# Product 4 of an up quad issued behind product 6 of the next quad

## The chip, the cores and the metric

The kernel runs on one core of one Trainium2 chip. The metric is the device time of one launch in microseconds (us). Three runs of the kernel before gave 1362.82, 1363.51 and 1364.30 us, a median of 1363.51 us.

## What is computed

Attention over 2 batches, 8 heads and 768 positions; then a dense layer pair with a sigmoid-weighted activation; then 8 experts, each a layer pair with a plain rectifier, mixed by weights that 8 rounds of row and column normalisation make even.

```python
def _moe_ref(x, w_in, w_out):            # x 1536x512, w_in 512x2048, w_out 2048x512
    h = x @ w_in
    g = h * (1.0 / (1.0 + np.exp(-h)))
    return g @ w_out

def _moe2_ref(x, w_gate, w1, w2):        # w1 8x512x1024, w2 8x1024x512
    logits = x @ w_gate
    P = np.exp(logits - logits.max())
    for _ in range(8):
        P /= P.sum(1, keepdims=True) + 1e-09
        P /= P.sum(0, keepdims=True) + 1e-09
        P *= N / E
    for e in range(E):
        out += P[:, e:e + 1] * (np.maximum(x @ w1[e], 0.0) @ w2[e])
```

## The kernel before

**Steps.** After attention, which ends about 104 us into the span, the work is 20 steps. A step is one batch (768 tokens) with one block of 1024 hidden columns. Steps 0 to 3 are the dense pair (two blocks for each of two batches, called the silu steps here), steps 4 to 19 are the 8 experts for batch 0 and then for batch 1 (the relu steps). Step 4 (`GATE`) also carries the gate: logits, their largest value, and the rounds of normalisation.

**Quads.** A step has four quads, i = 0 to 3, and then `down`. A quad makes two blocks of 128 hidden columns for both halves of the tokens out of seven products instead of eight: `RECIPE` names for each product the slot of the weights (a sum or difference of quarters) and the slot of the inputs. Each fp32 operand is split into a high and a low part (`up_h`, `up_l`, `xc_h`, `xc_l`), so that `multiply` issues six matmuls of 384 columns for each product: two halves of the depth times high-high, low-high and high-low. Names such as P6(3) below mean product 6 of quad 3.

**Banks.** P1 and P2 add up in a bank called a, P5 and P3 in c, P6 and P7 in b (two of each, used in turn by even and odd quads), and P4 in the single bank d. Between the products ScalarE copies partial sums: `keep_p1` copies a into b (P6 adds onto that copy, so `p6` waits for it), `keep_p5` copies c to SBUF, `keep_u2` copies b to SBUF after P6 (P7 waits for it), `keep_u3` copies b into d after P7 (P4 of that quad waits for it). VectorE adds the two remaining sums (`add12` after P3, `add22` after `keep_u3`).

**Order on TensorE before.** In a quad with i > 0: P1(i), P5(i), P4(i-1), P6(i), P2(i), P3(i), P7(i). Quad 0 has no P4, and P4(3) stands in `down`, in the first tile. P1(0) and P5(0) of the next step stand in the last tile of `down`.

**Order on ScalarE and VectorE.** Both work through queues that are written out by hand. ScalarE (`quad_work`): `keep_p1(i)`, `hidden22(i-1)`, `keep_p5(i)`, `hidden21(i-1)` (which waits for P4(i-1)), a rounding of new weights (`split_up` or `split_down`, L946, L956), `keep_u2(i)`, `hidden11(i)` (waits for P2), a second rounding, `hidden12(i)` (waits for `add12`), `keep_u3(i)`, a third rounding. VectorE: `hidden22(i-1)`, `hidden21(i-1)`, low part of the first rounding, `hidden11(i)`, low part of the second, `add12(i)`, `hidden12(i)`, `add22(i)`, low part of the third. In a relu step a hidden function is one instruction on each (L1013 and L1384); in a silu step it is one on ScalarE (L1019) and two on VectorE (L1390 and L1392).

**Weights just in time.** In quad i = 2 the weights of quad 3 are split, in three pieces (`PIECES`): slots 0 to 2, 3 and 4, 5 and 6. P1 uses slot 0, P5 slot 4, P4 slot 2, P6 slot 5, which is in the third piece: ScalarE rounds it behind `keep_u3(2)` and VectorE subtracts behind `add22(2)`. Quads 0, 1 and 2 of a step have theirs from the `down` before. In step 4, VectorE runs `rows_even` and `round_on` between the hidden functions of quads 2 and 3, each round waiting for a column sum of TensorE (`token_sums`), which waits for the step before it.

The counts that the waits on `product` use come from the table `made`, which lists the products in TensorE's order.

Of the kernel before, what the change touches and what calls it, by code (L numbers as in the profile page):

```python
# [29 lines left out]
def mixture_kernel(nc, qT, kT, v, vg, sizes, w_up, w_down, w_gate, out):  # L30
# [5 lines left out]
    NBLK, FP, _, _ = w_up.shape  # L36
# [18 lines left out]
    with ExitStack() as whole:  # L55
# [213 lines left out]

        made = {}  # L270
        for quad in range(QUADS):
            for name in ("P1", "P5", "P4", "P6", "P2", "P3", "P7"):
                if name != "P4":
                    made[quad, name] = len(made) + 1
                elif quad % FP:
                    made[quad - 1, name] = len(made) + 1
            if quad % FP == FP - 1:
                made[quad, "P4"] = len(made) + 1
# [38 lines left out]
        with nc.Block() as block:  # L317
# [241 lines left out]
            def _(pe):  # L559
# [127 lines left out]
                def multiply(quad, name, ps, add):  # L687
                    w, x = RECIPE[name]
                    s = quad // FP
                    pe.wait_ge(up_ready, len(PIECES) * quad + PIECE_OF[w] + 1)  # L690
                    if quad % FP == 0 and s in turns:
                        pe.wait_ge(xc_ready, SLOTS * turns.index(s) + x + 1)
                    n = 0
                    for k in range(2):
                        for a, b in ((up_h, xc_h), (up_h, xc_l), (up_l, xc_h)):
                            mm = nc.tensor.matmul(ps[:, 0:HALF], a[quad % UP_BUFS][:, w, k, :], b[x][:, k, :],  # L696
                                                  start=(n == 0 and not add), stop=(n == 5), skip_group_check=True)
                            n += 1
                    mm.then_inc(product, 1)

                def p1(s, i):
                    quad = s * FP + i
                    if i >= 2:
                        pe.wait_ge(hid_ready, 4 * (quad - 2) + 1)
                    elif s > 0:
                        pe.wait_ge(acc_ready, outs_before[s - 1] + 3 * i + 1)
                    multiply(quad, "P1", a_ps[i % 2], False)

                def p5(s, i):
                    quad = s * FP + i  # L710
                    if i >= 2:
                        pe.wait_ge(summed, 2 * (quad - 2) + 1)
                    elif s > 0:
                        pe.wait_ge(acc_ready, outs_before[s - 1] + 3 * i + 2)
                    multiply(quad, "P5", c_ps[i % 2], False)

                def p4(quad):
                    pe.wait_ge(kept, 4 * quad + 4)
                    multiply(quad, "P4", d_ps, True)

                def p6(s, i):
                    pe.wait_ge(kept, 4 * (s * FP + i) + 1)
                    multiply(s * FP + i, "P6", b_ps[i % 2], True)

                def p2(s, i):
                    multiply(s * FP + i, "P2", a_ps[i % 2], True)
# [58 lines left out]
                def turn_logits():  # L785
                    pe.wait_ge(gate_kept, 1)
                    place = ident[0:LOGITS, 0:32 * TB].rearrange("p (b r) -> p b r", r=32)[:, :, 0:E]
                    for n in range(WIDE):
                        mm = nc.tensor.matmul(g_ps[:, n * TB * E:(n + 1) * TB * E], logits_kept()[:, n * P:(n + 1) * P], place,
                                              start=True, stop=True)  # L790
                    mm.then_inc(gate_done, 1)
# [24 lines left out]
                def second_part():  # L816
                    for s in range(STEPS):
                        for i in range(FP):
                            if i > 0:
                                p1(s, i)  # L820
                                p5(s, i)
                            if s == GATE and i == 1:
                                turn_logits()
                            if i > 0:
                                p4(s * FP + i - 1)
                            if s == GATE and i == 2:
                                token_sums(0)
                            if s > 0 or i > 0:
                                p6(s, i)
                            if s == GATE and i == 1:  # L830
                                turn_top()
                            p2(s, i)
                            p3(s, i)
                            if s == GATE and i == 1:
                                spread_top()
                            p7(s, i)
                            if s == GATE and i == 0:
                                logits()
                            elif s == GATE and i > 1:
                                token_sums(i - 1)  # L840
                        down(s, {j: (lambda it=j + 2: token_sums(it)) for j in range(1, 6)} if s == GATE else {})
# [811 lines left out]
```

## Time and profile before

| | value |
|---|---|
| median of 3 runs | 1363.51 us |
| the profiled execution | 1364.54 us |
| its span, first to last instruction | 1363.0 us |
| mean granted TensorE clock | 0.998 |
| PE, weight load, VectorE, ScalarE, GpSimd busy | 99%, 90%, 58%, 46%, 24% |
| six L696 matmul groups and L761 groups on the chain that ended last | 38% and 38% of the span |

The busy shares are those of the whole span; matmuls overlap, so PE shows busy also where it only just keeps up. A matmul of 384 columns has a duration of 334 ns, yet the next one starts 0.17 us behind it, so a product of six takes 1.04 us. The same times recur in every relu step, one step being 62 us.

### The profile page before, as it was taken

The page shows a single profiled execution, that of the slowest core. Times are in us where ns is not written, and L with a number is a line of the kernel's source. Part 1 is how long each engine was busy: PE and PEld are TensorE (multiplying, and loading weights), DVE is VectorE, ACT ScalarE, POOL GpSimd, SP SyncE. Part 2 cuts the span into 40 slices and gives each one's busy share as a digit, 9 for nine tenths or more (in the row PEclk, how much of TensorE's full clock was granted, in tenths as well). Part 3 has the DMA queues.
Part 4 walks back from the last instruction along what each step waited for, and adds up shares of the span by engine and source line. Part 5 has one row for each costly group of instructions (what it writes and reads, how often), then busy time and mean ns, then how long its engine had stood idle before and what let it go on. Part 6 is the DMA issues. An engine that isn't in the chain of part 4 may idle for free.

```text
span 1363.0 us, 19886 instructions
## 1 busy us (share of the span) xinstructions
PE 1344.6 (99%) x7326; PEld 1223.8 (90%) x7326; DVE 794.2 (58%) x1444; ACT 620.9 (46%) x1323; POOL 325.6 (24%) x385
## 2 busy tenths in 40 slices
PE   7999999999999999999999999999999999999998
PEld 5779999999889898989898998989898998989896
DVE  6667476848486645546464647646464646455452
ACT  7786263526352533426262535435262535334250
POOL 6452303121311303030312302140313213040200
PEclk9999999999999999999999999999999999999999
DMA  7401212211212212121221212321212212131111
GB/s 240 142 4 55 86 47 85 79 53 57 74 49 85 87 38 93 47 78 47 85 78 55 78 62 70 102 92 47 77 58 82 77 61 91 36 93 47 62 32 63
DMA packets 48675, 98.73 MB, mean 72 GB/s; under 512 B 5313, under 2 KB 14529, under 8 KB 48577
## 3 DMA queue, kind: packets, MB, share of 16 engines
q1 hardware_dynamic: 48576, 97.42, 22.6%
q8 instruction: 62, 1.02, 0.3%
q14 instruction: 37, 0.29, 0.1%
HBM read 94.26 MB, written 3.15 MB: 71 GB/s over the span
## 4 chain that ended last, share of the span: by engine, by line
PE 90%; DVE 5%; ACT 3%; issue 1%; DMA 0%; DVEq 0%; ACTq 0%
PE bank L761 38%; PE bank L696 38%; PE bank L758 10%; ACT prob L876 1%; DVE hid_l L1392 1%; PE bank L572 1%; PE bank L585 1%; DVE hid_h L1390 1%; PE bank L605 1%; DVE up_l L1342 1%; ACT parts L1019 1%; PE bank L616 1%; DVE parts L1372 0%; DVE parts L1377 0%; PE bank L624 0%
## 5 line engine op out<-in xcount | busy, mean ns | idle before, releaser
L696 PE MATMUL bank<-xc_h,up_h 128*128 128x384 f32 x1120 | 375.9, 336 | 1.0 <-DVE up_l L1342 0.4
L696 PE MATMUL bank<-xc_h,up_l 128*128 128x384 f32 x1120 | 375.1, 335 | 0.0
L696 PE MATMUL bank<-xc_l,up_h 128*128 128x384 f32 x1120 | 374.9, 335 | 0.0
L761 PE MATMUL bank<-down_h,hid_l 128*128 128x512 f32 x768 | 299.7, 390 | 0.0
L761 PE MATMUL bank<-down_l,hid_h 128*128 128x512 f32 x768 | 299.6, 390 | 0.0
L761 PE MATMUL bank<-down_h,hid_h 128*128 128x512 f32 x768 | 299.4, 390 | 0.0
L482 POOL TENSOR_TENSOR up_raw<-up_raw 128x256 f32<-128x256 f32 x80 | 69.0, 863 | 896.2 <-DMA up_raw<-w_up 896.2
L1342 DVE TENSOR_TENSOR up_l<-up_raw,up_h 128x512 fp32r<-128x512 f32 (+1 forms) x234 | 200.8, 891 | 49.2 <-ACT up_h L946 49.0
L696 PEld LDWEIGHTS bank<-xc_h,up_h 128*128 128x128 f32 x1120 | 210.3, 188 | 6.8 <-issue 3.2
L696 PEld LDWEIGHTS bank<-xc_l,up_h 128*128 128x128 f32 x1120 | 210.3, 188 | 2.7
L696 PEld LDWEIGHTS bank<-xc_h,up_l 128*128 128x128 f32 x1120 | 210.3, 188 | 0.0
L946 ACT CAST up_h<-up_raw 128x512 fp32r<-128x512 f32 (+1 forms) x240 | 157.4, 687 | 67.8 <-POOL up_raw L487 64.3
L761 PEld LDWEIGHTS bank<-down_h,hid_l 128*128 128x128 f32 x768 | 144.1, 188 | 30.2
L761 PEld LDWEIGHTS bank<-down_l,hid_h 128*128 128x128 f32 x768 | 144.2, 188 | 28.0
L761 PEld LDWEIGHTS bank<-down_h,hid_h 128*128 128x128 f32 x768 | 144.2, 188 | 27.8
L1560 DVE SCALAR_TENSOR_TENSOR x_sb<-bank,mix,x_sb 128x512 f32<-128x512 f32 x84 | 60.0, 751 | 178.1 <-PE bank L761 178.1
L979 ACT COPY bank<-bank 128x384 f32<-128x384 f32 x80 | 37.1, 464 | 269.4 <-PE bank L696 269.4
L956 ACT CAST down_h<-down_raw 128x512 fp32r<-128x512 f32 x160 | 98.9, 618 | 95.5 <-PE bank L761 70.8
L1347 DVE TENSOR_TENSOR down_l<-down_raw,down_h 128x512 fp32r<-128x512 f32 x160 | 125.2, 785 | 27.4 <-ACT down_h L956 27.3
L1384 DVE SCALAR_TENSOR_TENSOR hid_l<-bank,hid_h 128x384 fp32r<-128x384 f32 x128 | 71.3, 558 | 114.0 <-ACT hid_h L1013 114.0
L1384 DVE SCALAR_TENSOR_TENSOR hid_l<-parts,hid_h 128x384 fp32r<-128x384 f32 x128 | 76.1, 595 | 71.2 <-ACT hid_h L1013 69.0
L1013 ACT ACTIVATE hid_h<-parts 128x384 fp32r<-128x384 f32 x128 | 67.1, 524 | 98.8 <-DVE parts L1372 78.4
(119 smaller groups left out, 1484.2 us busy)
## 6 DMA issues: line engine op xcount, KB each, us to landing
up_raw<-w_up SPq DMA_DIRECT2D x80, 512.0 KB, 3.5
down_raw<-w_down SPq DMA_DIRECT2D x160, 256.0 KB, 2.7
k_sb<-kT SPq DMA_DIRECT2D x12, 288.0 KB, 4.5
q_sb<-qT SPq DMA_DIRECT2D x12, 256.0 KB, 3.9
v_sb<-v SPq DMA_DIRECT2D x12, 256.0 KB, 4.5
out<-x_sb SPq DMA_DIRECT2D x12, 256.0 KB, 2.7
vg_sb<-vg SPq DMA_DIRECT2D x2, 256.0 KB, 5.4
nraw<-sizes SPq DMA_DIRECT2D x1, 2.0 KB, 2.8
```

The source lines that it names most:

```text
L482: nc.gpsimd.tensor_tensor(w[4], w[3], w[2], ALU.add).then_inc(up_summed, 1)
L696: mm = nc.tensor.matmul(ps[:, 0:HALF], a[quad % UP_BUFS][:, w, k, :], b[x][:, k, :], start=(n == 0 and not add), stop=(n == 5), skip_group ...
L758: mm = nc.tensor.matmul(ps[:, 0:HALF], w[a][:, t // 2 * P:t // 2 * P + P], x[b][:, t % 2, :], start=start, stop=stop)
L761: mm = nc.tensor.matmul(ps[:], x[a][:, t // 3, t % 3 * P:t % 3 * P + P], w[b], start=start, stop=stop)
L946: nc.scalar.copy(up_h[quad % UP_BUFS][:, lo:hi, :, :], up_raw[:, quad % RAWS, lo:hi, :, :]).then_inc(up_h_ready, 1)
L956: nc.scalar.copy(down_h[:, tile % DOWN_BUFS, :], down_raw[:, tile % RAWS, :]).then_inc(down_h_ready, 1)
L979: nc.scalar.copy(b_ps[i % 2][:, 0:HALF], a_ps[i % 2][:, 0:HALF]).then_inc(kept, 1)
L1013: nc.scalar.activation(hid_h[:, f, half, :], src, ACT.Relu).then_inc(hid_h_ready, 1)
L1342: nc.vector.tensor_tensor(up_l[quad % UP_BUFS][:, lo:hi, :, :], up_raw[:, quad % RAWS, lo:hi, :, :], up_h[quad % UP_BUFS][:, lo:hi, :, :]. ...
L1347: nc.vector.tensor_tensor(down_l[:, tile % DOWN_BUFS, :], down_raw[:, tile % RAWS, :], down_h[:, tile % DOWN_BUFS, :].bitcast(F32), ALU.su ...
L1384: nc.vector.scalar_tensor_tensor(low, src, 0.0, h.bitcast(F32), ALU.max, ALU.subtract).then_inc(hid_ready, 1)
L1560: nc.vector.scalar_tensor_tensor(acc(c, t), part, weight, acc(c, t), ALU.mult, ALU.add).then_inc(acc_ready, 1)
```

## The change

In `second_part`, the call of `p4` for the quad before moves from in front of `p6` to behind it. The order of a quad with i > 0 becomes P1(i), P5(i), P6(i), P4(i-1), P2(i), P3(i), P7(i). The table `made` is changed in the same way, so every wait on a product still means the same product. In step 4, `token_sums(0)` stood behind P4(1) and now stands directly behind P5(2); `turn_top` stood behind P6(1) and now has P4(0) between.

```diff
-            for name in ("P1", "P5", "P4", "P6", "P2", "P3", "P7"):
+            for name in ("P1", "P5", "P6", "P4", "P2", "P3", "P7"):
...
-                            if i > 0:
-                                p4(s * FP + i - 1)
                             if s == GATE and i == 2:
                                 token_sums(0)
                             if s > 0 or i > 0:
                                 p6(s, i)
+                            if i > 0:
+                                p4(s * FP + i - 1)
```

The queues of ScalarE, VectorE, GpSimd and SyncE hold the same instructions in the same order as before. On TensorE, quad 3 of step 5 (every step from 1 on has this pattern, apart from the numbers of the weight buffers): the first of the six matmuls of P1, P5, P4, P6, P2, P3 and P7 before. bank4 is d, bank3 is b, bank5 is a, bank6 is c; up_h1 holds the weights of quad 2, up_h2 those of quad 3.

```order
L696 MATMUL bank5<-xc_h0_62,up_h2_82 128x384 [waits up_ready,hid_ready]
...
L696 MATMUL bank6<-xc_h1_63,up_h2_82 128x384 [waits up_ready,summed]
...
L696 MATMUL bank4<-xc_h6_75,up_h1_107 128x384 [waits up_ready,kept]
...
L696 MATMUL bank3<-xc_h2_64,up_h2_82 128x384 [waits up_ready,kept]
...
L696 MATMUL bank5<-xc_h3_65,up_h2_82 128x384 [waits up_ready]
```

The same place of the changed kernel, on TensorE:

```order
L696 MATMUL bank5<-xc_h0_62,up_h2_82 128x384 [waits up_ready,hid_ready]
...
L696 MATMUL bank6<-xc_h1_63,up_h2_82 128x384 [waits up_ready,summed]
...
L696 MATMUL bank3<-xc_h2_64,up_h2_82 128x384 [waits up_ready,kept]
...
L696 MATMUL bank4<-xc_h6_75,up_h1_107 128x384 [waits up_ready,kept]
...
L696 MATMUL bank5<-xc_h3_65,up_h2_82 128x384 [waits up_ready]
```

P6(3), which reads the third piece of new weights and adds onto the copy of P1, has moved up by one product, and P4(2), for which `hidden21(2)` waits, has moved down by one.

On TensorE, quad 2 of step 4, where the first column sum (L803) stands. Before:

```order
L696 MATMUL bank1<-xc_h1_63,up_h0_72 128x384 [waits up_ready,summed]
...
L696 MATMUL bank4<-xc_h6_75,up_h2_82 128x384 [waits up_ready,kept]
...
L803 MATMUL bank7<-mix_58,ones_54 128x96 [waits gate_step]
L696 MATMUL bank2<-xc_h2_64,up_h0_72 128x384 [waits up_ready,kept]
...
L696 MATMUL bank0<-xc_h3_65,up_h0_72 128x384 [waits up_ready]
```

And in the changed kernel:

```order
L696 MATMUL bank1<-xc_h1_63,up_h0_72 128x384 [waits up_ready,summed]
...
L803 MATMUL bank7<-mix_58,ones_54 128x96 [waits gate_step]
L696 MATMUL bank2<-xc_h2_64,up_h0_72 128x384 [waits up_ready,kept]
...
L696 MATMUL bank4<-xc_h6_75,up_h2_82 128x384 [waits up_ready,kept]
...
L696 MATMUL bank0<-xc_h3_65,up_h0_72 128x384 [waits up_ready]
```

The column sum now has P5(2) in front of it in place of P4(1), and P4(1) (bank4) stands behind both the sum and P6(2).

## Rows read from the trace of the kernel before

**Rows 1.** The page's busy times: us (share of the span) and instructions.

```profile
PE 1344.6 (99%) x7326; PEld 1223.8 (90%) x7326; DVE 794.2 (58%) x1444; ACT 620.9 (46%) x1323; POOL 325.6 (24%) x385
```

**Rows 2.** Waits of PE's weight loads: us in total, times, longest us.

```profile
PEld bank L696 <- ACT bank L1008: 0.7, 2, 0.4
```

**Rows 3.** The chain that ended last: start us, us, what, instructions.

```profile
233.36 9.37 PE bank L696 x54
...
259.78 1.56 PE bank L758 x9
...
429.68 26.02 PE bank L696 x150
...
1297.30 26.02 PE bank L696 x150
```

**Rows 4.** Timeline of PE, step 6: first matmul of P4(2). Start, us, what.

```profile
512.31 0.33 PE L696 MATMUL bank<-xc_h,up_h 128*128 128x384 f32 x1
```

**Rows 5.** Timeline of ScalarE, step 6, quads 2 and 3; brackets: idle before, releaser.

```profile
504.19 0.46 ACT L979 COPY bank<-bank 128x384 f32<-128x384 f32 x1
...
506.27 0.49 ACT L1013 ACTIVATE hid_h<-bank 128x384 fp32r<-128x384 f32 x1 [0.47 <-PE bank L696]
506.65 0.83 ACT L946 CAST up_h<-up_raw 128x768 fp32r<-128x768 f32 x1
...
510.57 0.53 ACT L1013 ACTIVATE hid_h<-parts 128x384 fp32r<-128x384 f32 x1 [1.22 <-DVE parts L1372]
...
511.41 0.61 ACT L946 CAST up_h<-up_raw 128x512 fp32r<-128x512 f32 x1
511.93 0.47 ACT L979 COPY bank<-bank 128x384 f32<-128x384 f32 x1
```

**Rows 6.** Timeline of VectorE, step 6, quad 2.

```profile
507.51 0.96 DVE L1342 TENSOR_TENSOR up_l<-up_raw,up_h 128x768 fp32r<-128x768 f32 x1 [0.17 <-ACT up_h L946]
508.87 0.56 DVE L1384 SCALAR_TENSOR_TENSOR hid_l<-bank,hid_h 128x384 fp32r<-128x384 f32 x1 [0.40 <-ACT hid_h L1013]
509.38 0.69 DVE L1342 TENSOR_TENSOR up_l<-up_raw,up_h 128x512 fp32r<-128x512 f32 x1
509.99 0.55 DVE L1372 TENSOR_TENSOR parts<-parts,bank 128x384 f32<-128x384 f32 x1
...
511.60 0.55 DVE L1377 TENSOR_TENSOR parts<-parts,bank 128x384 f32<-128x384 f32 x1
512.07 0.69 DVE L1342 TENSOR_TENSOR up_l<-up_raw,up_h 128x512 fp32r<-128x512 f32 x1
```

**Rows 7.** Timeline of step 2 (silu): ScalarE, VectorE, then the weight load of P6(3).

```profile
246.18 0.44 ACT L979 COPY bank<-bank 128x384 f32<-128x384 f32 x1
...
250.56 0.36 DVE L1390 CAST hid_h<-parts 128x384 fp32r<-128x384 f32 x1
...
251.44 0.69 DVE L1342 TENSOR_TENSOR up_l<-up_raw,up_h 128x512 fp32r<-128x512 f32 x1
...
254.51 0.69 DVE L1342 TENSOR_TENSOR up_l<-up_raw,up_h 128x512 fp32r<-128x512 f32 x1
...
255.32 0.19 PEld L696 LDWEIGHTS bank<-xc_h,up_h 128*128 128x128 f32 x1 [0.43 <-issue]
```

**Rows 8.** Timeline of step 4: VectorE in quad 2, then PE at P6(3).

```profile
379.32 0.26 DVE L1428 TENSOR_TENSOR mix<-mix,tsum 128x96 f32<-128x96 f32 x1
...
380.62 0.25 DVE L1433 TENSOR_REDUCE esum<-bank 128x8 f32<-128x96 f32 x1
...
382.89 0.96 DVE L1342 TENSOR_TENSOR up_l<-up_raw,up_h 128x768 fp32r<-128x768 f32 x1
...
387.75 0.41 PE L696 MATMUL bank<-xc_h,up_h 128*128 128x384 f32 x1
```

**Rows 9.** Stretches: us, busy PE, PEld, DVE, ACT, POOL, clock, DMA share, GB/s.

```profile
20.00:24.00 4.00, 4.00 (x34) 3.05 (x31) 2.82 (x11) 1.61 (x6) 0.00 (x0) 0.68 0.86 307
...
372.00:376.00 4.00, 3.69 (x22) 3.32 (x20) 2.83 (x6) 1.77 (x5) 0.00 (x0) 1.00 0.22 66
```

## The prediction

> **What bounds the kernel now.** I read the busy times, the waits, the chain that ended last, and the timelines of ScalarE and VectorE around one quad. TensorE is busy 99% of the span [rows 1] and the chain is nearly all its own. In the relu steps it waits for nothing between P6(0) and `down`: 25 products in 26.02 us, 1.041 us each, and the same 26.02 us in all 15 relu steps behind step 4 [rows 3]. So the kernel can hardly gain, and a wait that TensorE gets is a loss in full, since there is no slack in which it could catch up. The question is how close behind TensorE the others already run. In the silu steps they are too close: from P6(0) to `down` step 2 takes 259.78 - 233.36 = 26.42 us [rows 3], 0.40 more for the same 25 products, and the wait lies at P6(3): the last piece of weights was ready at 254.51 + 0.69 = 255.20 and the weight load of P6(3) began at 255.32 [rows 7]. P6(3) is product 22 from P6(0), due at 233.20 + 21 x 1.041 = 255.06 (the chain's pieces begin 0.16 behind the first matmul's start); it ran as if begun at 255.46. So from the end of a VectorE subtraction to the product's start I count **0.25 us**; for a ScalarE copy 0.2, an estimate just under it.
>
> **The change part by part.** Nothing is added or taken away: 60 products P4 of quads 0 to 2 change places with 60 products P6. By itself that is worth 0. What counts is that each P6 is asked for 1.04 us sooner and each P4 is delivered 1.04 us later.
>
> *P6 sooner.* P6(i) waits for `keep_p1(i)` and, in quad 3, for the third piece of weights. Step 6: P4(2) begins at 512.31 [rows 4], and that is now P6(3)'s place. The copy of P1 ends at 511.93 + 0.47 = 512.40 [rows 5], the third piece at 512.07 + 0.69 = 512.76 [rows 6]; with 0.25 that is 513.01, against P6(3)'s present place of 512.31 + 1.04 = 513.35. So there was 0.34 us of slack, and 1.04 is taken: even if nothing else moved, TensorE would wait 0.70 us in each relu step.
>
> *P4 later.* On ScalarE `hidden21(1)` waits for P4(1), and everything behind it in the queue waits with it, up to the very piece of weights that P6(3) needs. This is the larger half, so I follow it in step 6. P4(1) began at 512.31 - 7 x 1.04 = 505.03 and `hidden21` at 506.27 [rows 5], 1.24 later. P4(1) now begins at 506.07 and `hidden21` at 507.31. Behind it (start to start 0.38) the rounding of piece one begins at 507.69 and ends 0.83 later, 508.52 [rows 5]. VectorE's subtraction of that piece begins 0.03 behind, 508.55 (before 507.51), and takes 0.96 [rows 6]. VectorE had idle time here, 0.17 and 0.40 us, and it is used up: `hidden11(2)` begins at 509.5, not 508.87. From there the spacing is as before: +0.51 to piece two (510.0), +0.61 to `add12(2)` (510.6, before 509.99), and from `add12` through ScalarE's `hidden12` and `add22` to the third piece 512.07 - 509.99 = 2.08 [rows 6], so 512.67. ScalarE's rounding of the third piece, 511.41 + 0.60 + 0.61 = 512.62 [rows 5], is just in time. The piece is ready at 513.36 and P6(3) begins at 513.61, **1.30 us** behind its place of 512.31. The copy of P1 (ending at 513.00) is hidden below this. Behind P6(3) stand P4, P2, P3, P7 and `down` as before, and nothing there is late: `keep_u3(3)` and the sums follow P7 as before.
>
> *Quads 1 and 2 of a relu step.* P6(2) takes the place 505.03. The copy of P1 ended at 504.19 + 0.46 = 504.65 [rows 5]. By the same reckoning the later P4(0) delays `add12(1)` by 0.23 (VectorE and ScalarE had more idle time there), which moves the copy's end to about 504.8; with 0.2 it is due at 505.0. No wait, with no margin: 0, at most 0.15. Quad 1 has its copy 0.38 us before, no wait. 15 steps x 1.30 = **19.5 us** (with 0.15 more each, 21.8; without any shift of the queues 15 x 0.70 = 10.5).
>
> *Silu steps 1 to 3.* A hidden function here holds VectorE 251.44 - 250.56 = 0.88 us [rows 7] where a relu step has 0.51 [rows 6], 0.37 more. Three lie on the chain from P4(1) to the third piece (`hidden21`, `hidden11`, `hidden12`), less 0.2 that the first hides behind ScalarE's rounding: 0.9 more than the relu chain. That chain was 513.61 - 506.07 = 7.54 us from P4(1)'s start to P6(3)'s; here 8.44, against six products (6.24) that TensorE has for it: 2.2 us of wait. In quad 2 the copy of P1 ends at 246.18 + 0.44 = 246.62 [rows 7], and the place that P6(2) gets is 246.72 (seven products before 254.00, where P4(2) stands); moved by about 0.5 by the longer queue of quad 1 it costs with quad 1's 0.1 about 0.6. Sum 2.2 + 0.6 - 0.4 (the present wait) = 2.4; three steps, **7.2 us**.
>
> *Step 0* has the silu queues. Two waits for `keep_u3`, 0.7 us together [rows 2], stand at P4(0) and P4(1); P4 is now late enough for them to vanish, but P6(1) and P6(2), in the same places, wait for `keep_p1`, the next instruction of ScalarE behind `keep_u3`, some 0.4 to 0.9 later. I take **2.5 us**, as a silu step.
>
> *Step 4.* The first column sum waits for the mix weights, ready at 379.32 + 0.26 = 379.58 [rows 8]; it stands one product earlier and waits for them 1.04 longer, so P6(2) begins about 380.0 and P4(1) at 381.05, where before it was over at 379.3. `hidden21(1)` on VectorE is then done at 383.5, and only behind it comes the round, 382.89 - 380.62 = 2.27 us of small instructions [rows 8]: piece one begins at about 385.6, not 382.89, 2.7 later. From there to P6(3) it is 513.61 - 508.55 = 5.06 us as in step 6, so 390.6. Before, P6(3) stood at 387.75 [rows 8] (0.1 more for its slow first matmul) with four products to the end of the quads; now five: 2.7 + 1.04 = **3.7 us**.
>
> **Sum.** 19.5 + 7.2 + 2.5 + 3.7 = 32.9 us. On the profiled execution, 1364.54 us (span 1363.0), that is 1397.4; on the median of the runs, 1363.51, it is 1396.4. I give 1396.5.
>
> The Trainium skill, Perfetto Trace Analysis, section Optimizing Tensor Performance, wants independent groups of matmuls to rotate through the banks of PSUM, so that the copying out of one overlaps the next. By it this change is good: P4 gets further from the `keep_u3` that fills its bank, and P6 further from P7 on bank b. What it would be worth is the first rival below.
>
> **The rivals.** *Not slower: the copies before P4 were the tight ones.* The waits for L1008 are the only ones of this kind [rows 2]; with P4 behind P6 they go, 0.7 us, and if ScalarE had P1's copy and the third piece early enough, the time would be 1362.8, within the noise or slightly faster. It decides where the third piece ends 1.29 us or more before P6(3)'s present place; the rows say 513.35 - 512.76 = 0.59. Only if the semaphore came well ahead of the recorded end would this hold, and the wait in [rows 7] says it comes after.
>
> *Only the bare slack is lost.* If the queues swallowed the later P4 (idle of 0.47 and 1.22 us before `hidden21` and `hidden12` [rows 5] speaks for it), a relu step would lose 0.70: 10.5, silu steps 1.04 each, 3.1, step 0 1, step 4 about 2: 16.6 us, 1380. Against it: the 1.22 is a wait for VectorE, whose own queue is full behind 508.87.
>
> *A longer chain.* P6(2) waits too in the relu steps (0.15 each, 2.3 us), the overlaps of ScalarE's instructions shrink by a few hundredths each, and step 0 and step 4 lose one more microsecond each: 1400 to 1404.
>
> *The clock falls.* After the thin start of attention TensorE was granted 0.68 of its clock for 4 us [rows 9], a mix of 1.2 and 2.4 GHz; that cost about 1.3 us. Once in each of 20 steps it would add 26 us: 1422. Against it: the stretch of step 4 in which PE idles 0.31 us has the full clock [rows 9], and the waits here are 1.3 to 2.2 us amid dense work. The Trainium skill, TensorE: Matmul & The Clock Gate, section HAM oscillation, describes such a fall at gaps that recur in each tile; no run so far shows it for gaps of this size.
>
> That the change doesn't do what it says is excluded by the order of the instructions: P6 stands in front in all 60 places.
>
> **How the numbers follow.** Forecast (1388 to 1400) 0.74; bare slack only 0.09; longer chain 0.09; clock 0.03; not slower 0.05. The range goes down to the bare slack and up to the longer chain: 1380 to 1404. A change under 0.2% (2.7 us) can't be told from none here. Faster by more: 0.01; within it: 0.04; slower by more: 0.95.
>
> **What would show it.** In the changed profile the waits of PE for VectorE's L1342 appear about 20 times, 1.2 to 1.3 us in the relu steps and some 2 in the silu steps, all at P6(3); the 26.02 us stretches become 27.3; the idle time of 0.17 and 0.40 on VectorE in quad 2 is gone; ScalarE's waits for L979 copies show at P6(1) or P6(2) in the silu steps only; the clock stays at 1.00. Wrong would be: the third piece ending at the same distance behind P7(2) as before (then the queues swallowed it), waits at P7 or in `down`, or a granted clock under 0.98.

## The result and the profile after

The changed kernel takes **1398.22 us** (median of 4 runs, 1397.66 to 1399.44) against 1363.53 us of the kernel before on the same chip (4 runs, 1362.82 to 1364.30): ratio 1.0254, 95% interval 1.0241 to 1.0266. The profiled execution took 1398.52 us, its span 1397.0 us.

The page: the busy times, and the group of first matmuls of the products (busy us, mean ns of one, idle time before them and what ended most of it).

```profile
PE 1353.5 (97%) x7326; PEld 1225.5 (88%) x7326; DVE 790.3 (57%) x1444; ACT 613.2 (44%) x1323; POOL 322.8 (23%) x385
...
L696 PE MATMUL bank<-xc_h,up_h 128*128 128x384 f32 x1120 | 379.7, 339 | 25.3 <-DVE up_l L1342 23.1
```

TensorE does the same 7326 matmuls as in [rows 1] and is no longer at 99%. The idle time in front of L696 is 25.3 us, 23.1 of it ended by VectorE's subtraction of weights. The waits of PE (us in total, times, longest):

```profile
PE bank L696 <- DVE up_l L1342: 23.1, 21, 1.8
...
PE bank L696 <- ACT bank L979: 1.8, 5, 0.7
```

The same view for the weight loads, where the kernel before had [rows 2]:

```profile
PEld bank L696 <- ACT bank L979: 31.7, 25, 2.1
...
PEld bank L696 <- ACT bank L1008: 1.4, 3, 0.5
```

The two views name different causes for the same stalls: the matmul's says the third piece of weights, the weight load's says ScalarE's copy of P1. Which of them it is, the experiments have to say. The chain that ended last, in the step that answers to the one of [rows 4 to 6] (start us, us, what):

```profile
509.11 15.66 PE bank L696 x90
530.90 5.44 PE bank L696 x30
536.34 2.08 PE bank L761 x9
```

From P6(0) to `down` it is 536.34 - 509.11 = 27.23 us, where [rows 3] had 26.02, and the chain leaves TensorE behind P4(1), 15 products from P6(0), and comes back to it at P6(3): between them it runs through `hidden21(1)` and what stands behind it on ScalarE and VectorE. Step lengths, from one P1(0) to the next in this view, and how they stand to the forecast:

| | before | after | more | forecast |
|---|---|---|---|---|
| step 0 (from its first P1) | 68.96 | 72.74 | 3.78 | 2.5 |
| silu steps 1, 2, 3 | 62.92, 62.93, 62.91 | 65.66, 67.21, 65.62 | 2.74, 4.28, 2.71 = 9.7 | 7.2 |
| step 4 | 70.07 | 73.80 | 3.73 | 3.7 |
| relu steps 5 to 19 | 61.97 | 63.17 | 15 x 1.20 = 18.0 | 19.5 |
| attention, in this execution | | | -0.97 | 0 |
| sum | | | 34.2 (spans: 34.0) | 32.9 |

Step 19 has no P1(0) behind it; up to the end of the kernel it is only 0.95 us longer, which is the 0.2 between the sum and the spans.

ScalarE and VectorE around quad 2 of that step (start us, us, what, idle time before and what ended it), ScalarE first, then VectorE:

```profile
524.80 0.49 ACT L1013 ACTIVATE hid_h<-bank 128x384 fp32r<-128x384 f32 x1 [1.30 <-PE bank L696]
525.18 0.83 ACT L946 CAST up_h<-up_raw 128x768 fp32r<-128x768 f32 x1
...
529.92 0.47 ACT L979 COPY bank<-bank 128x384 f32<-128x384 f32 x1
```

```profile
526.04 0.96 DVE L1342 TENSOR_TENSOR up_l<-up_raw,up_h 128x768 fp32r<-128x768 f32 x1 [0.16 <-ACT up_h L946]
526.92 0.55 DVE L1384 SCALAR_TENSOR_TENSOR hid_l<-bank,hid_h 128x384 fp32r<-128x384 f32 x1
527.39 0.68 DVE L1342 TENSOR_TENSOR up_l<-up_raw,up_h 128x512 fp32r<-128x512 f32 x1
527.99 0.55 DVE L1372 TENSOR_TENSOR parts<-parts,bank 128x384 f32<-128x384 f32 x1
...
530.07 0.68 DVE L1342 TENSOR_TENSOR up_l<-up_raw,up_h 128x512 fp32r<-128x512 f32 x1
```

And PE at P6(3):

```profile
529.63 0.34 PE L696 MATMUL bank<-xc_h,up_l 128*128 128x384 f32 x1
530.90 0.41 PE L696 MATMUL bank<-xc_h,up_h 128*128 128x384 f32 x1 [0.93 <-DVE up_l L1342]
```

P6(3)'s place is 529.63 + 0.17 = 529.80. The copy of P1 ends at 529.92 + 0.47 = 530.39, the third piece at 530.07 + 0.68 = 530.75, and P6(3) begins at 530.90, 1.10 late; its slow first matmul brings the loss to 1.20. The bracket reads 0.93 only because it counts from the end of the matmul before, not from the place.

### The profile page after: what moved, and what is told of

It reads as the page before. It is cut to its first block, busy times and chain, and to the rows that moved or that the text cites. A ratio compares the mean times of both kernels' runs of the same rounds, so it can differ in the third digit from the quotient of the medians.

```text
span 1397.0 us, 19886 instructions
## 1 busy us (share of the span) xinstructions
PE 1353.5 (97%) x7326; PEld 1225.5 (88%) x7326; DVE 790.3 (57%) x1444; ACT 613.2 (44%) x1323; POOL 322.8 (23%) x385
## 4 chain that ended last, share of the span: by engine, by line
PE 83%; DVE 10%; ACT 5%; issue 2%; DMA 0%; ACTq 0%; DVEq 0%
PE bank L761 37%; PE bank L696 32%; PE bank L758 9%; DVE up_l L1342 3%; PE bank L572 1%; DVE hid_l L1384 1%; PE bank L585 1%; DVE parts L1372 1%; ACT up_h L946 1%; ACT prob L876 1%; PE bank L605 1%; DVE hid_l L1392 1%; DVE hid_h L1390 1%; ACT hid_h L1013 1%; DVE parts L1377 1%
## 5 line engine op out<-in xcount | busy, mean ns | idle before, releaser
L696 PE MATMUL bank<-xc_h,up_h 128*128 128x384 f32 x1120 | 379.7, 339 | 25.3 <-DVE up_l L1342 23.1
L696 PE MATMUL bank<-xc_h,up_l 128*128 128x384 f32 x1120 | 376.7, 336 | 0.0
L696 PE MATMUL bank<-xc_l,up_h 128*128 128x384 f32 x1120 | 376.6, 336 | 0.0
L696 PEld LDWEIGHTS bank<-xc_h,up_h 128*128 128x128 f32 x1120 | 211.3, 189 | 38.4 <-ACT bank L979 31.7
L696 PEld LDWEIGHTS bank<-xc_l,up_h 128*128 128x128 f32 x1120 | 211.2, 189 | 2.7
L696 PEld LDWEIGHTS bank<-xc_h,up_l 128*128 128x128 f32 x1120 | 211.3, 189 | 0.0
L979 ACT COPY bank<-bank 128x384 f32<-128x384 f32 x80 | 36.7, 459 | 269.8 <-PE bank L696 269.8
L1384 DVE SCALAR_TENSOR_TENSOR hid_l<-parts,hid_h 128x384 fp32r<-128x384 f32 x128 | 72.6, 567 | 71.2 <-ACT hid_h L1013 69.1
```

Of the source, the lines that this page charges most:

```text
L979: nc.scalar.copy(b_ps[i % 2][:, 0:HALF], a_ps[i % 2][:, 0:HALF]).then_inc(kept, 1)
L1384: nc.vector.scalar_tensor_tensor(low, src, 0.0, h.bitcast(F32), ALU.max, ALU.subtract).then_inc(hid_ready, 1)
```

## The experiments

The theory: P6(3) waits for the third piece of weights; that piece is late by the slack that the new order takes (0.70 us in a relu step) and by the queues of ScalarE and VectorE, which now stand behind the later P4(1) (the rest). The rivals: it waits for the copy of P1; or the shift of the queues is swallowed; or the new order is good and something else costs. The lengths of the relu steps in one kernel agree within 0.06 us, unless said otherwise. Lines of these kernels can stand a few lower or higher than in the listing.

| | median us | ratio [95%] | relu step | silu steps 1 to 3 | step 4 |
|---|---|---|---|---|---|
| after | 1398.22 | 1.0254 [1.0241, 1.0266] | 63.17 | 65.66, 67.21, 65.62 | 73.80 |
| e1_q12 | 1373.95 | 1.0076 [1.0059, 1.0093] | 62.15 | 64.19, 64.16, 64.17 | 72.76 |
| e2_q3 | 1379.79 | 1.0121 [1.0104, 1.0138] | 62.67 | 64.41, 63.95, 63.94 | 71.08 |
| e3_piece0 | 1385.17 | 1.0159 [1.0142, 1.0176] | 62.67 | 65.07, 65.07, 65.10 | 72.95 |
| e4_early | 1372.13 | 1.0059 [1.0042, 1.0076] | 62.00 | 64.59, 64.62, 64.57 | 72.12 |
| e5_before_early | 1367.81 | 1.0026 [1.0015, 1.0037] | 61.97 | 63.81, 63.81, 63.78 | 71.08 |
| e6_p4_later | 1446.27 | 1.0605 [1.0589, 1.0622] | 65.37 | 69.04, 69.71, 70.61 | 76.13 |
| e7_copy_first | 1404.60 | 1.0299 [1.0283, 1.0315] | 63.55 | 65.70, 67.35, 65.72 | 74.20 |
| e8_sums_late | 1400.26 (one run) | | 63.19 | 67.28, 65.70, 67.22 | 73.84 |
| e9_before_gap | 1362.64 | 0.9988 [0.9979, 0.9997] | 61.97 | 62.75, 63.01, 62.63 | 69.71 |
| e10_gap | 1377.91 | 1.0095 [1.0080, 1.0111] | 62.23 | 64.61, 64.97, 65.12 | 72.87 |
| e11b_piece_twice | 1417.18 | 1.0388 [1.0372, 1.0404] | 63.93 | 68.08, 68.14, 68.06 | 74.54 |
| e12b_piece_thrice | 1437.67 | 1.0538 [1.0522, 1.0554] | 64.65; 3 of 66.0 to 66.2 | 68.87, 68.66, 69.23 | 76.86 |

### The change in parts: quads 1 and 2 alone, quad 3 alone

```diff
-for name in ("P1", "P5", "P4", "P6", "P2", "P3", "P7"):
+for name in (("P1", "P5", "P6", "P4", "P2", "P3", "P7") if quad % FP in (1, 2) else ("P1", "P5", "P4", "P6", "P2", "P3", "P7")):
...
-                            if i > 0:
+                            if i > 0 and i not in (1, 2):
                                 p4(s * FP + i - 1)
...
                                 p6(s, i)
+                            if i in (1, 2):
+                                p4(s * FP + i - 1)
```

> P4 stands behind P6 in quads 1 and 2 only; quad 3 keeps the order of before. My theory (the later P4(1) shifts the queues of ScalarE and VectorE up to the third piece of quad 3's weights): P6(3) has its old place, 1.04 us later than in the changed kernel where it waited 1.20, so 0.16 us of wait in each of 15 relu steps, 2.4 us; silu steps 1.4 each, 4.2; steps 0 and 4 about 2.7 each: 12 us over before, about 1375.5, and VectorE's third piece in quad 2 of a relu step still ends about 0.5 us later than before. Rival (the copy of P1, named by the waits of the weight loads, is what costs, and only in quad 3): nothing in the relu steps, about 5 us from the silu steps, 1368 to 1369.

With quads 1 and 2 alone the queues shift, but P6(3) keeps its old place. A relu step grows by 0.18 us: of the shift of 0.50 (1.20 - 0.70) the old slack of 0.34 covers all but 0.16. In the relu steps nobody pays for P6(2) in its new place, as the prediction took it: in the changed kernel the waits of PE's matmuls for L979 are five, all before the relu steps.

e2_q3 is the same edit with `(3,)` in place of `(1, 2)`:

> P4(2) stands behind P6(3) in quad 3 only; quads 1 and 2 keep the order of before, so nothing shifts before P6(3). My theory: only the bare slack is lost, 0.70 us in each of 15 relu steps (10.5), 1.04 in the silu steps (3.1), about 1 each in steps 0 and 4: 15.7 us over before, about 1379. Rival (the copy of P1): it ended at 512.40 for a place of 512.31, 0.3 us in each of 20 steps, 6 us, about 1369.5.

The relu step grows by 62.67 - 61.97 = **0.70 us**, the bare slack exactly. Alone the two halves give 0.70 and 0.18, together 1.20: the 0.34 of slack can be used once only.

### The shift of the queues: the first piece ahead of `hidden21`

The changed kernel with the first piece of new weights in front of `hidden21(1)` on both engines, so that this piece doesn't wait for P4(1). ScalarE's edit is shown; VectorE's is the same.

```diff
+                    if i == 2:
+                        split_up(quad + 1, 0)
                     if i > 0:
                         hidden21(s, i - 1)
                     if i == 2:
-                        split_up(quad + 1, 0)
+                        pass
```

> The changed kernel, but in quad 2 ScalarE rounds and VectorE subtracts the first piece of quad 3's weights before hidden21(1) instead of behind it. My theory: the chain from P4(1) to the third piece loses the 0.83 and 0.96 us of the first piece, hidden11(2) is back at its old time, and a relu step waits 0.70 us instead of 1.20; silu steps about 1.8, step 0 about 2, step 4 about 2.8: 21 us over before, about 1384. Rival (the copy of P1): ScalarE's queue in front of the copy in quad 3 is the same work, the time stays at 1398.

The relu step falls from 63.17 to 62.67: the 0.50 of the shift is gone and the 0.70 stays. With this the two terms of the relu sum stand apart, each measured by a run of its own.

### All pieces earlier, in the kernel after and before

Pieces one and two stand ahead of `hidden21(1)`, the third in the place of the second, on both engines (ScalarE's edit is shown).

```diff
+                    if i == 2:
+                        split_up(quad + 1, 0)
+                        split_up(quad + 1, 1)
                     if i > 0:
                         hidden21(s, i - 1)
...
-                        split_up(quad + 1, 1)
+                        split_up(quad + 1, 2)
...
-                        split_up(quad + 1, 2)
+                        pass
```

> The changed kernel, but in quad 2 pieces one and two are split before hidden21(1) and the third piece takes the place of the second, before hidden12(2), on ScalarE and VectorE. My theory: in a relu step the third piece is ready 2 us before P6(3) asks for it and nothing waits, step length back at 61.97 us; silu steps keep 0.6 us at P6(2) and lose their old 0.4 at P6(3); steps 0 and 4 about 2 each: 3 to 6 us over before, about 1368. Rival (the copy of P1 is the wait): the waits at P6(3) stay near 1.2 us, 1385 to 1398.

The relu step comes back to 62.00, 0.03 above before, with the new order of products in place. So in the relu steps the order itself costs nothing; the lateness of the weights does. The time missed the forecast by 4 us: the silu steps kept 1.7 us each. The same edit of the kernel before helps to see why:

> The kernel before (P4 in front of P6) with the earlier pieces of the run before: pieces one and two before hidden21(1), the third in the place of the second. My theory: the 0.4 us waits at P6(3) in silu steps 1 to 3, 0.6 in step 0 and 0.3 in step 4 go, nothing else changes: 2 us less, about 1361.5. Rival: the earlier pieces push hidden21(1) and with it other work, and the time is 1363.5 or more.

It made the kernel slower by 0.26%. VectorE in quad 2 of silu step 2:

```profile
252.97 0.69 DVE L1345 TENSOR_TENSOR up_l<-up_raw,up_h 128x512 fp32r<-128x512 f32 x1
253.57 0.55 DVE L1375 TENSOR_TENSOR parts<-parts,bank 128x384 f32<-128x384 f32 x1
```

Here the third piece stands in front of `add12(2)` (L1375), on which `hidden12`, `keep_u3` and then P4(2) hang. A silu step has no room there: the wait of 0.4 at P6(3) moved to P4(2), which loses 0.5 us. That alone would leave the time about as it was. The 0.9 us by which a silu step grew is lost at P4(3), in `down`: it waits 0.62 us for `keep_u3(3)`, since VectorE takes 0.90 and 0.98 us twice over for what takes it 0.36 and 0.56 elsewhere:

```profile
258.53 0.98 DVE L1395 TENSOR_TENSOR hid_l<-parts,hid_h 128x384 fp32r<-128x384 f32 x1
259.43 0.90 DVE L1393 CAST hid_h<-parts 128x384 fp32r<-128x384 f32 x1
```

GpSimd's sums of the next weights run beside these rows (below, "GpSimd beside VectorE"). They wait for the next load into the buffer that the third piece was read from (`next_up` waits for that subtraction), and in most silu steps of these kernels they begin 3.5 to 3.8 us behind the end of its subtraction. So a third piece that is done sooner also brings the sums sooner, onto VectorE's hidden functions. In e4_early P4(3) waits 0.54 us, behind rows stretched in the same way. (Step 4 grew by 1.0 us in e5_before_early: its P1(3) comes 0.7 later, and the rest is at P4(2) and P4(3).) How much of the silu steps' loss would stay without the sums, no run shows.

### The third piece in VectorE's gap

Behind `add12` VectorE idles 0.59 us while ScalarE does its half of `hidden12` (the kernel before, step 6):

```profile
511.13 0.56 DVE L1384 SCALAR_TENSOR_TENSOR hid_l<-parts,hid_h 128x384 fp32r<-128x384 f32 x1 [0.59 <-ACT hid_h L1013]
```

ScalarE rounds the third piece right behind the second, and VectorE subtracts it in that gap:

```diff
                         split_up(quad + 1, 1)
+                        split_up(quad + 1, 2)
...
                     add12(s, i)
+                    if i == 2:
+                        split_up(quad + 1, 2)
                     hidden12(s, i)
...
                     add22(s, i)
-                    if i == 2:
-                        split_up(quad + 1, 2)
```

In the changed kernel:

> The changed kernel with the same move of the third piece. Theory (the third piece is the last of two things that P6(3) waits for; the copy of P1 by ScalarE is just below it, ready about 0.3 us before): a relu step falls from 63.17 to 62.2 to 62.35, the wait that is left is one for the copy of P1 (L979), and the kernel takes 1376 to 1380 us. Rival (the copy of P1 is itself the limit): relu step stays at 63.0 or more, 1395 to 1398 us.

The relu step is 62.23, 0.26 above before, and the waits that are left name the other input. First PE's waits, then its weight loads':

```profile
PE bank L696 <- ACT bank L979: 3.7, 10, 0.6
...
PE bank L696 <- DVE up_l L1341: 0.6, 1, 0.6
```

```profile
PEld bank L696 <- ACT bank L979: 10.7, 25, 0.9
```

The copy of P1, in step 6 of e10_gap:

```profile
522.49 0.44 ACT L979 COPY bank<-bank 128x384 f32<-128x384 f32 x1
```

It ends at 522.93, and P6(3), whose place was 522.88, begins at 522.98. So the copy is a second limit, here worth 0.26 us. In the changed kernel it is worth more, because ScalarE's rounding of the third piece still stands in front of it: there it ended 0.59 behind the place (530.39 for 529.80), against 0.05 here, so my estimate of what it would cost there without the third piece is 0.26 + 0.54 = 0.80 us. No run has that case; it lies below the 1.20 that the third piece costs. The weight load's view of after, which put all 31.7 us down to the copy, named an input that was 0.36 us earlier than the one that decided.

In the silu steps the gain is small: P4(3) waits 0.53, 0.92 and 1.09 us, and VectorE's rows in front of it are stretched beside GpSimd's sums as in e5_before_early. In the kernel before:

> The kernel before, with only the third piece of weights moved: ScalarE rounds it right behind the second piece, and VectorE subtracts it between add12(2) and hidden12(2), where it idles 0.59 us. Theory (the third piece is what P6(3) waits for in the silu steps; in the gap it delays nothing): the waits at P6(3) go, 0.4 us in each of steps 1 to 3, about 0.6 in step 0 and 0.3 in step 4: 1361.5 us, ratio 0.9985. Relu steps stay at 61.97. Rival (hidden12(2) starts 0.1 us later and in the silu queues this moves keep_u3 and P4(2)): no gain, 1363.5 to 1365.

VectorE in silu step 2, and the chain in silu step 1:

```profile
249.53 0.55 DVE L1371 TENSOR_TENSOR parts<-parts,bank 128x384 f32<-128x384 f32 x1
250.00 0.69 DVE L1341 TENSOR_TENSOR up_l<-up_raw,up_h 128x512 fp32r<-128x512 f32 x1
```

```profile
168.11 23.93 PE bank L696 x138
193.33 0.87 issue
195.73 1.31 PE bank L696 x6
```

The wait at P6(3) is gone: from P6(0) the chain is one piece of 138 matmuls, 23.93 us, past P6(3). A part of it is back at P4(3), which starts at 195.73 behind `keep_u3(3)` and in step 2 waits 0.29 us. It isn't the rival's P4(2), which waits nowhere. In step 2 the sums begin 1.7 us sooner behind P1(3) than before, and VectorE's cast and subtraction in front of `add12(3)` take 0.91 and 0.98 us, beside them. So the silu steps gain only 0.17, -0.08 and 0.28, step 4 gains 0.36 and step 0 1.06 (67.90 for 68.96). The runs say 0.9988 [0.9979, 0.9997], 1.7 us between the medians: the only one of these kernels that comes out under the kernel before, but narrowly, and by less than the 0.2% that I had called the limit of what can be told.

### Which of the two it is, from the other side

The copy of P1 for quad 3 in front of the third rounding on ScalarE, in the changed kernel:

```diff
                         keep_p1(s, i)
+                    if i == 3:
+                        split_up(quad, 2)
                     if i > 0:
                         hidden22(s, i - 1)
...
-                    if i == 2:
-                        split_up(quad + 1, 2)
-                    elif s == 0 and i == 1:
+                    if s == 0 and i == 1:
```

> The changed kernel, but on ScalarE the copy keep_p1(3) stands before the rounding of the third piece instead of behind it; VectorE's queue is unchanged. My theory (the third piece is what P6(3) waits for): the piece is ready about 0.5 us later, in 20 steps 8 to 10 us, about 1407. Rival (the copy): it ends 0.5 us earlier, about 1388.

The copy comes 0.5 us sooner and the relu step grows by 0.38, since the third piece is 0.34 later. In the silu steps, where VectorE's queue and not ScalarE's rounding sets the third piece, it grows by 0.04 to 0.14 only; so the total is 1404.6 us and not 1407.

The third piece subtracted twice, and three times, by VectorE:

```diff
+                    if quad % FP == 3 and piece == 2:
+                        for again in range(1):
+                            nc.vector.tensor_tensor(up_l[...], up_raw[...], up_h[...], ALU.subtract).then_inc(again_step, 1)
+                            dve.wait_ge(again_step, (quad // FP) + again + 1)
```

> The changed kernel with VectorE's subtraction of the third piece done twice in each step, one behind the other (0.61 us and about 0.06 for a semaphore). Theory (third piece is the last): every step grows by 0.67 us, a relu step to 63.84, 20 x 0.67 = 13.4 us, 1411.6 us, with a wait of about 1.8 us at P6(3) in each relu step. If a wait of that size brings the clock down each time, as it did in two steps of the changed kernel for about 1.5 us, 15 x 1.5 us more: 1434 us. Rival (P6(3) waits for the copy of P1): nothing changes, 1398 us.

> The same with the subtraction done three times: each step 1.34 us longer than in the changed kernel, a relu step 64.5, waits of about 2.5 us at P6(3). Theory (third piece is the last, waits under 3 us leave the clock at 2.4 GHz): 1425 us. With the clock falling in every step for 1.5 us more: 1455 us. Rival (copy of P1): 1398 us.

The relu step grows by 63.93 - 63.17 = 0.76 and 64.65 - 63.17 = 1.48, 0.74 to 0.76 for each subtraction (I had taken 0.67; the subtractions start 0.72 apart, so the step through a semaphore costs 0.11, not 0.06). Every added microsecond on the third piece is a microsecond of the step. With e4_early and e10_gap, where the loss went with the piece, that settles which input is waited for. Both runs are longer than that in each of 20 steps gives, 1417.2 for 1413.4 us and 1437.7 for 1427.8: the clock, below.

### P4 two places later

```diff
-            for name in ("P1", "P5", "P6", "P4", "P2", "P3", "P7"):
+            for name in ("P1", "P5", "P6", "P2", "P4", "P3", "P7"):
```

with the call of `p4` behind `p2` in the same way.

> P4(i-1) stands one product later still, behind P2(i); P6 where the changed kernel has it. My theory (half of the loss is hidden21 waiting for P4 with the weights behind it): another 1.04 us at P6(3) in every step, and keep_u2, which stands behind hidden21 on ScalarE, now holds up P7 by 0.7 us in quad 1 and some in quad 3: 20 to 35 us over the changed kernel, 1418 to 1433. Rival (P6 waits for the copy of P1, which does not depend on P4): 1398 to 1400.

Right in direction, short by 13 us, and not by the way that I gave: a relu step is 2.20 us longer than after, but P6(3) waits only 0.13 longer (1.06 for 0.93) and not 1.04, since TensorE has already lost time in quads 1 and 2, where a third thing comes too late. PE's waits at P7(2) and P6(3) of step 6:

```profile
545.27 0.44 PE L696 MATMUL bank<-xc_h,up_h 128*128 128x384 f32 x1 [0.64 <-ACT parts L995]
...
549.72 0.41 PE L696 MATMUL bank<-xc_h,up_h 128*128 128x384 f32 x1 [1.06 <-DVE up_l L1342]
```

`keep_u2` (L995), for which P7 waits, stands behind `hidden21` and the rounding on ScalarE, and with P4 later still TensorE runs into it at P7(1) (0.42 us) and P7(2) (0.64). The clock also fell in three steps. P4 as late as possible isn't a direction to go on in.

### GpSimd beside VectorE

One wait of the silu steps stands in no step of the prediction. VectorE in step 1 of the changed kernel; the first pair of rows is undisturbed:

```profile
199.38 0.36 DVE L1390 CAST hid_h<-parts 128x384 fp32r<-128x384 f32 x1 [2.08 <-ACT parts L1019]
199.78 0.56 DVE L1392 TENSOR_TENSOR hid_l<-parts,hid_h 128x384 fp32r<-128x384 f32 x1
200.43 0.73 DVE L1390 CAST hid_h<-parts 128x384 fp32r<-128x384 f32 x1
201.19 0.97 DVE L1392 TENSOR_TENSOR hid_l<-parts,hid_h 128x384 fp32r<-128x384 f32 x1
202.09 0.54 DVE L1372 TENSOR_TENSOR parts<-parts,bank 128x384 f32<-128x384 f32 x1
```

GpSimd's sums of weights (four, from 199.91) run beside them:

```profile
199.91 1.02 POOL L482 TENSOR_TENSOR up_raw<-up_raw 128x256 f32<-128x256 f32 x1 [38.67 <-DMA up_raw<-w_up]
```

The two take 0.78 us more than the pair before; `add12(3)` and `keep_u3(3)` are late by it, and P4(3) waits:

```profile
203.62 0.44 PE L696 MATMUL bank<-xc_h,up_h 128*128 128x384 f32 x1
```

By the matmul before it, which began at 203.17, it was due at 203.34: 0.28, and 0.11 for its slow first pair. In the kernel before the sums begin later against VectorE's work, and of the rows that they stretch none stands ahead of `add12(3)`. The experiment, on the changed kernel, holds GpSimd's sums for quad 1 of the next step back until P4(3) is done:

```diff
+                    if quad % FP == 1 and 1 < quad // FP <= GATE:
+                        pool.wait_ge(product, made[quad - 2, "P4"])
```

> The changed kernel, but in steps 1 to 3 GpSimd begins its sums for the next step's quad 1 only when P4(3) is done, so that they no longer lie beside VectorE's hidden functions of quad 3. My theory: those take 0.36 and 0.56 us instead of 0.73 and 0.97, the waits at P4(3) for keep_u3 (0.2 to 0.3 us) in steps 1 to 3 go, about 0.9 us in all, 1397.3. Rival: the slow instructions stay slow, and the time too.

This kernel ran once, and its clock fell in three of steps 0 to 3 where it fell in two of after, so its total says little; the rows decide. The stretching went from this place, and the wait at P4(3) with it. The cost came back elsewhere: in step 2 of e8_sums_late the sums run beside the last hidden function, and the first matmul of the next block waits for that. VectorE, then PE:

```profile
271.84 2.02 DVE L1394 TENSOR_TENSOR hid_l<-parts,hid_h 128x384 fp32r<-128x384 f32 x2
```

```profile
273.91 0.44 PE L760 MATMUL bank<-hid_h,down_h 128*128 128x384 f32 x1 [0.29 <-DVE hid_l L1394]
```

The step without a fall of the clock is 65.70, as long as in after (65.62 to 65.66). The contention is shown; that it can be got rid of is not.

By how much a row is stretched can be counted. In the silu steps of all these kernels 204 rows of the cast (L1390 in after) and the subtraction (L1392) start while a sum runs. 199 of them are longer than the usual 0.36 or 0.56 us by what is left of that sum, less 0.14 to 0.15 us; for L1392 at 201.19 that is 0.56 left and 0.42 more. Four had under 0.15 us left and lost nothing; one, in e3_piece0, fits neither. The 42 rows that started just ahead of a sum kept their 0.36 and 0.56.

The Trainium skill, SBUF — State Buffer, section "SBUF: two separate sides", says that VectorE and GpSimd share a pair of ports, that a VectorE operation with two inputs in SBUF or in a two-port mode contends for it, and that whichever starts first has the pair for its whole instruction while the other is blocked. The trace agrees, in who is stretched (L1392 reads two tiles in SBUF; L1372, which reads a bank, takes its 0.54 beside a sum), in the part of the first to start, and in how long the other waits, but for the 0.14 us. That the cast L1390, with its one input, runs in a two-port mode is what its stretching would say; no row shows the mode.

## Why the prediction was right, and where it was not

**What bounds the kernel: right.** TensorE can't catch up, so each wait at P6(3) came through whole, in every step.

**The bare slack, 0.70 us: right** (e2_q3: 0.70).

**The shift of the queues, 0.60: 0.50.** The walk through the queues held row by row, but for one sign: I had said that the idle times of 0.17 and 0.40 on VectorE would both go, and 0.16 stays in front of the first subtraction, as my own sum had it (it moved that subtraction by the full 1.04). The rest: `hidden21(1)` 1.24 behind P4(1) (524.80 against 529.80 - 6 x 1.04 = 523.56), the first rounding 0.38 behind that, the subtraction 0.03 behind its end, the gap of 0.40 on VectorE used up, and 2.08 from `add12(2)` to the third piece (527.99 to 530.07). Short of it fell two small steps. I let `hidden11(2)` begin when the first piece ended, 0.95 behind it; VectorE overlaps them, 0.88. And to the second piece it is 0.47, not 0.51, since nothing waits any more. Together 0.10 a step, 15 x 0.10 = 1.5 us too much. With a queue that is full to the brim the distance is start to start, as two neighbours without idle time show it, and never duration plus a bit.

**Quads 1 and 2 of a relu step, 0: right.** No wait of a matmul for L979 in any relu step.

**Silu steps, 2.4: 2.7, and a fall of the clock.** P6(3) begins at 196.50 in step 1; seven products and 0.1 behind P6(2)'s first matmul at 187.07 would be 194.4. With its slow first matmul that costs 2.1, for 2.2 forecast. P6(2) costs 0.5 and P6(1) 0.1, for 0.6, and the 0.4 of before goes, as forecast. What is missing is P4(3), 0.39, from the GpSimd sums: a collision that no view of one engine's queue shows. P4(3) stands in `down`, where I had named a wait as a sign of being wrong; in the silu steps that sign came up, and the sentence that nothing behind P6(3) is late, which I had worked out for a relu step, did not hold for them.

**Step 0, 2.5: 2.4 of waits,** at P6(1), P6(2) and P6(3); less 0.3 at the start of `down`, and 1.7 more from the clock. The waits, as forecast:

```profile
111.49 0.44 PE L696 MATMUL bank<-xc_h,up_h 128*128 128x384 f32 x1 [0.50 <-ACT bank L979]
...
119.71 0.44 PE L696 MATMUL bank<-xc_h,up_h 128*128 128x384 f32 x1 [0.67 <-ACT bank L979]
...
129.15 0.41 PE L696 MATMUL bank<-xc_h,up_h 128*128 128x384 f32 x1 [1.78 <-DVE up_l L1342]
```

**Step 4, 3.7: right, with its path.** The last instruction of the round and the first piece behind it on VectorE, then P6(3):

```profile
397.86 0.26 DVE L1428 TENSOR_TENSOR mix<-mix,tsum 128x96 f32<-128x96 f32 x1
398.15 0.96 DVE L1342 TENSOR_TENSOR up_l<-up_raw,up_h 128x768 fp32r<-128x768 f32 x1
```

```profile
403.00 0.41 PE L696 MATMUL bank<-xc_h,up_h 128*128 128x384 f32 x1 [1.37 <-DVE up_l L1342]
```

The piece begins 398.15 - 368.62 = 29.53 us behind P1(0) of the step, where [rows 8] had 382.89 - 356.08 = 26.81: 2.72 later, for 2.7. That piece also holds up P1(3) by 0.62 us, where I had all the waits at P6(3). It costs nothing on top, since P6(3), two products on, waits for a piece that comes later still.

**The clock: wrong.** I gave its fall a chance only as a matter of all 20 steps or none, and wrote that the clock would stay at 1.00. It fell in step 0 and in step 2, for 3.2 us in all. The sum came out at 32.9 for 34.0 because the relu steps' 1.5 too much, the 1.0 of attention and the 0.3 at `down` stood against this and against the 1.0 of P4(3): the total is nearer than its parts, and that is luck.

**The rivals.** That the copies before P4 were the tight ones fell at once. The idea of the Trainium skill, Perfetto Trace Analysis, section Optimizing Tensor Performance (rotate the banks so that copying out overlaps), is about what the reordering did for `keep_u3` and bank b: the waits for L1008 were 0.7 us in two places before and are 1.4 in three after, so no gain of it shows here. The waits of step 0 at P4(0) and P4(1) did go, as forecast; P6(1) and P6(2) in the same places wait longer, for L979, and the three of after stand at P4(3).

## What to carry to other kernels

When an engine at 99% gets a product in an earlier place, look at each input of that product and take its ready time from the row, not the engine's share: the slack is the distance to the old place, and what the new order makes later upstream comes on top, but slack can be spent only once. Follow the queue behind the instruction that now waits, start to start, until it reaches the input again. When two inputs are close, the profile names one and the other stands right behind it; only taking one away shows the second. And where a buffer is filled again as soon as its last reader is done, an earlier reader brings the next filling sooner: look at what that will run beside.

## What the runs showed of the hardware

**The clock fell at waits of TensorE below 2 us, but not at all of them.** Windows of the kernel after (us, busy us and instructions of PE, weight load, VectorE, ScalarE, GpSimd; granted clock; share of DMA; GB/s):

```profile
129.00:132.00 3.00, 2.85 (x11) 2.88 (x12) 0.91 (x3) 0.33 (x1) 0.00 (x0) 0.64 0.00 0
262.00:266.00 4.00, 3.83 (x14) 3.86 (x15) 0.93 (x3) 0.61 (x2) 0.25 (x1) 0.62 0.37 131
528.00:534.00 6.00, 5.07 (x30) 4.78 (x29) 2.94 (x7) 3.39 (x8) 0.00 (x0) 1.00 0.25 87
```

A share of 0.62 is a mix of 1.2 and 2.4 GHz; a matmul there takes 0.52 us, the next one 0.32 behind, for 0.33 and 0.17. The wait in front was the same in steps 1, 2 and 3, and only in step 2 was the clock lost:

```profile
196.50 0.41 PE L696 MATMUL bank<-xc_h,up_h 128*128 128x384 f32 x1 [1.77 <-DVE up_l L1342]
...
262.17 0.41 PE L696 MATMUL bank<-xc_h,up_h 128*128 128x384 f32 x1 [1.78 <-DVE up_l L1342]
...
263.57 0.52 PE L696 MATMUL bank<-xc_h,up_h 128*128 128x384 f32 x1
```

The count over the kernels, by the wait at P6(3). Relu steps: 15 waits of 0.93 us (after), 15 of 1.30 (e7_copy_first) and 15 of 1.66 (e11b_piece_twice) without a fall; of 15 waits of 2.39 (e12b_piece_thrice) three brought one. Steps 0 to 3: of 16 waits of 1.77 to 1.79 nine (two each in after, e6_p4_later and e7_copy_first, three in e8_sums_late), of four of 2.5 (e11b_piece_twice) and of four of 3.2 (e12b_piece_thrice) all. Step 4: none at 2.11 (e11b_piece_twice), one at 2.83 (e12b_piece_thrice). So neither of the two cases that I had written ahead of the last two runs holds, no fall under 3 us or a fall each time. In e12b_piece_thrice, two relu steps with the same wait; the chain, then windows:

```profile
549.00 5.46 PE bank L697 x30
...
613.65 6.85 PE bank L697 x30
```

```profile
549.00:552.00 3.00, 3.00 (x17) 3.00 (x18) 0.42 (x2) 0.62 (x2) 0.00 (x0) 1.00 0.56 175
613.00:617.00 4.00, 3.35 (x11) 3.38 (x12) 0.98 (x2) 0.00 (x0) 0.00 (x0) 0.57 0.48 133
```

A fall costs 6.85 - 5.46 = 1.4 us on the 30 matmuls behind it, 1.4 to 1.7 in the lengths of steps. From step to step of one kernel the waits agree to 0.02 us and the falls do not, so the length of one wait doesn't decide alone. Waits of 1.8 us in the silu steps, which have a second wait at P6(2) before them, did more than those of 2.39 in the relu steps; what else decides stays open here. The Trainium skill, TensorE: Matmul & The Clock Gate, section HAM oscillation, describes falls at idle gaps that recur between groups of matmuls. These runs agree that a wait amid dense work can bring one, and show that the same wait may or may not.

**GpSimd's additions stretch VectorE's two-input subtraction and its cast** when these start while an addition runs, by what is left of it less 0.14 us (0.42 for most rows of L1392, up to 0.58 for the cast), and not when VectorE starts first. Moving the additions moves the cost.
